# Cutting POOL's subtractions for the low parts of the weights into pieces of 256 columns

## The chip, the cores and the metric

The kernel runs on one core of one Trainium2 chip. The time is that of one execution on the device, in microseconds (us). A core has five engines that run their own instruction streams and meet at semaphores: TensorE (PE: matmuls, with weight loads counted beside them), VectorE (DVE), ScalarE (ACT), GpSimd (POOL) and SyncE (SP, which here only issues DMAs).

## What is computed

Attention with a window and four sink positions, then two mixtures of experts in a row. Cut to what matters here:

```python
x = attention(q, k, v)                      # 3072 tokens, 512 wide
# first mixture: each token goes to its best expert
h = np.maximum(x[mask] @ w1[e], 0.0)        # 512 -> 1024
out[mask] = gate_w[mask, None] * (h @ w2[e])
# second mixture: each expert takes 384 tokens, by a greedy assignment over all scores
for idx in np.argsort(-logits.flatten()):
    tok, e = idx // E, idx % E
    if assigned[tok] < 0 and counts[e] < cap: assigned[tok] = e; counts[e] += 1
h = np.maximum(x[mask] @ w1[e], 0.0)
out[mask] = h @ w2[e]
```

There are 8 experts in each mixture, with their own w1 (512 x 1024) and w2 (1024 x 512).

## The kernel before

Every product runs as three products of rounded numbers: each operand is split in a high part (ACT's cast to fp32r) and a low part (operand minus high part), and TensorE adds high x high, low x high and high x low. So each weight matrix of an expert needs a cast by ACT and a subtraction. Both work on a matrix in four parts (WP = 4) of 128 x 1024; w1 in parts of one row block each, w2 in parts of two.

The first mixture (324 to 728 us) runs over tiles of 128 tokens, ordered by expert; three experts have tokens here. DVE makes the low parts of w1 (low_w1, line 1413), POOL those of w2 (low_w2, line 523). POOL also gathers each tile's rows by an indirect DMA (line 515), two tiles ahead. For expert 0 POOL's order is: gather tiles 0 and 1, four w2 parts, gather tile 2. At a change of expert ACT casts w1, then scales the last tile's result, then casts w2, and POOL's four w2 parts stand in its queue ahead of the next gather. TensorE's up product waits for w1's parts one after the other.

The second mixture (728 us to the end) runs over 8 experts of 384 tokens. Here POOL makes all low parts. Its queue for expert k, written out by hand:

- for each of the eight blocks f of the hidden layer, low_h (line 586), which waits for ACT's two relus of that block; after each of the first four also one part of w2 (low_w2)
- the gather of the next expert's tokens (line 561, three indirect DMAs); w1 parts 0 and 1 of the next expert (low_w1, line 575), w1 part 2; the scatter of result tile 0 (line 592); low_x 0 (line 581), w1 part 3, low_x 1; a wait until the scatter has landed, scatter 1, low_x 2; the same wait, scatter 2, and a last wait.

TensorE computes the up product of block f (line 922 to 924) when ACT is done with block f-2 (two PSUM banks), and ACT's block f needs POOL's low_h of block f-2 (two h32 buffers). After eight blocks come three tiles of the down product (line 938 to 940), with the transposes of the next expert's gathered rows among them (line 753). The next expert's up product starts with a wait for all three low_x (line 912) and for w1's parts (line 921).

The second routing (the greedy assignment, rewritten as a search over thresholds) runs two experts ahead: DVE prepares `passed` (line 1509), TensorE counts with many small matmuls (line 833) that are placed among the products of experts 0 to 4 at fixed places, the first of them right behind an expert's first three products; experts 5 to 7 have none of it but a few leftovers of slots. DVE keeps one operand of nearly all its routing instructions in PSUM.

SP loads the raw w2 of the next expert when w2's four low parts are done, and raw w1 when those of w1 are.

Of the kernel before, what the change touches and what calls it, by code (L numbers as in the profile page):

```python
# [5 lines left out]
ALU = mybir.AluOpType  # L6
ACT = mybir.ActivationFunctionType
AX = mybir.AxisListType
F32 = mybir.dt.float32
# [9 lines left out]
def attention_then_two_moes(nc, qT, kT, v, mod_id, mod_bias, wg1, w1a, w2a, wg2, w1b, w2b, out):  # L19
# [5 lines left out]
    DM, E = wg1.shape  # L25
    F = w1a.shape[2]
    DC, FC = DM // P, F // P
# [24 lines left out]
    with ctx:  # L52
        def sb(name, shape, dt=F32):
            return ctx.enter_context(nc.sbuf_tensor("sb_" + name, shape, dt))
# [4 lines left out]
        def sem(name):  # L59
            return ctx.enter_context(nc.semaphore(name))  # L60
# [136 lines left out]
        w1h, w1l = sb("w1h", [P, DC, F], F32R), sb("w1l", [P, DC, F], F32R)  # L197
        w2h, w2l = sb("w2h", [P, FC, DM], F32R), sb("w2l", [P, FC, DM], F32R)
# [90 lines left out]
        w1_hi, w1_lo = [sem(f"w1_hi{m}") for m in range(2)], [sem(f"w1_lo{m}") for m in range(2)]  # L289
        w2_hi, w2_lo = [sem(f"w2_hi{m}") for m in range(2)], [sem(f"w2_lo{m}") for m in range(2)]  # L290
# [14 lines left out]
        WP = 4  # L305
        raw1, raw2 = w1_raw, w2_raw

        def w1_part(w, p):
            return w[:, p]

        def w2_part(w, p):
            return w[:, p * (FC // WP):(p + 1) * (FC // WP)]
# [110 lines left out]
        def _(pool):  # L423
# [96 lines left out]

            def low_w2(m, j, p):
                pool.wait_ge(w2_hi[m], j * WP + p + 1)
                pool.tensor_tensor(w2_part(w2l, p), w2_part(raw2, p), w2_part(w2h, p).bitcast(F32), ALU.subtract  # L523
                                   ).then_inc(w2_lo[m], 1)

            gather_x(0)
            gather_x(1)
            for p in range(WP):
                low_w2(0, 0, p)
            used = used_experts(pool)  # L530
            with pool.Fori(0, used) as e:
                first, end = order_of(pool, e, FIRST, END)
                with pool.Fori(first, end) as t:
                    gather_x(t + 2)
                first, end = order_of(pool, e + 1, FIRST, END)
                with pool.If(end > first):
                    for p in range(WP):
                        low_w2(0, e + 1, p)
# [33 lines left out]

            def low_w1(k, p):
                pool.wait_ge(w1_hi[1], k * WP + p + 1)
                pool.tensor_tensor(w1_part(w1l, p), w1_part(raw1, p), w1_part(w1h, p).bitcast(F32), ALU.subtract  # L575
                                   ).then_inc(w1_lo[1], 1)

            def low_x(k, i):
                pool.wait_ge(x2_hi, k * CT + i + 2)
# [21 lines left out]
            for p in range(WP):  # L601
                low_w1(0, p)
# [5 lines left out]
            def expert(k, a, last):  # L608

                for f in range(FC):  # L610
                    low_h(k, f)
                    if f < WP:
                        low_w2(1, k, f)

                if not last:
                    gather(k + 1, 1 - a)
                    low_w1(k + 1, 0)
                    low_w1(k + 1, 1)
                    keep_tokens(k + 1, 1 - a)
                    low_w1(k + 1, 2)  # L620
                scatter(k, a, 0)
                if not last:
                    low_x(k + 1, 0)
                    low_w1(k + 1, 3)
                    low_x(k + 1, 1)
                landed(k, 0)
                scatter(k, a, 1)
                if not last:
                    low_x(k + 1, 2)
                landed(k, 1)  # L630
                scatter(k, a, 2)
                landed(k, 2)
# [1024 lines left out]
```

## Time and profile before

| | |
|---|---|
| timed runs (3) | 1199.67, 1208.88, 1211.93 us; median 1208.88 |
| profiled execution | 1197.59 us, of it 1195.8 us span |
| busy | PE 1043.4, DVE 492.8, ACT 459.8, POOL 489.2 us |
| granted TensorE clock, mean | 0.925 of full speed |

The profile is of one execution. It has, among others, a view of groups of instructions by line, a timeline of single instructions, stretches with each engine's busy time and the granted TensorE clock, the waits, and the chain of work that ended last. In a timeline row the bracket tells how long the engine was idle before the instruction and what ended that. A matmul's duration is modelled and overlaps the next; the distance of two starts is what one costs. The full clock is 2.4 GHz and stands as 1.00; 0.50 is 1.2 GHz.

### The profile page before, as it was taken

What the parts mean: (1) busy time and instruction counts of PE and PEld (TensorE: products, weight loads), DVE (VectorE), ACT (ScalarE), POOL (GpSimd) and SP (SyncE); (2) the same over time, 40 slices, a digit from 0 to 9 for tenths busy, and PEclk for the clock granted to TensorE, in tenths of its full rate; (3) what the DMA queues carried; (4) which work ended last, traced back from release to release, by engine and by line L of the source; (5) the groups of instructions that cost most, each with busy time, mean ns of one, the idle gap of its engine ahead of it and who ended that gap; (6) DMA issues with size and microseconds to landing.
All of it is one profiled execution on the core that took longest, in us unless ns stands there. A gap on an engine that the chain in (4) does not pass through costs nothing.

```text
span 1195.8 us, 22961 instructions
## 1 busy us (share of the span) xinstructions
PE 1043.4 (87%) x7189; PEld 881.2 (74%) x7190; DVE 492.8 (41%) x1577; ACT 459.8 (38%) x1094; POOL 489.2 (41%) x453
## 2 busy tenths in 40 slices
PE   5999999999159999989999985259999999998796
PEld 4888888888147888878888874248777787887685
DVE  4566666665641111141112235864546455541000
ACT  4666666665032222242222240114243333433541
POOL 6443443442032000023000130226776766878782
PEclk9999999999569999999999997559898999988998
DMA  7545545642153111114111110322332333324300
GB/s 199 138 112 144 141 115 138 151 114 72 54 188 110 39 35 36 43 35 167 43 35 35 36 34 18 142 97 85 111 99 98 122 137 130 98 97 166 125 27 27
DMA packets 57148, 113.54 MB, mean 95 GB/s; under 512 B 6416, under 2 KB 22800, under 8 KB 57104
## 3 DMA queue, kind: packets, MB, share of 16 engines
q1 hardware_dynamic: 51024, 92.95, 25.6%
q0 software_dynamic: 6080, 19.98, 5.2%
q8 instruction: 31, 0.51, 0.2%
q14 instruction: 13, 0.11, 0.0%
HBM read 91.34 MB, written 21.57 MB: 94 GB/s over the span
## 4 chain that ended last, share of the span: by engine, by line
PE 48%; POOL 15%; issue 14%; DVE 8%; DMA 7%; ACT 4%; DVEq 2%; POOLq 1%; another core or an unknown queue 0%; SPq 0%; ACTq 0%
DMA out<-sb_rows_out,sb_tokens_at 5%; POOL sb_w2l L523 5%; PE ps_bank L792 4%; POOL sb_hl L586 4%; PE ps_bank L794 4%; PE ps_bank L793 4%; PE ps_bank L776 4%; PE ps_bank L774 4%; PE ps_bank L775 4%; PE ps_bank L677 3%; PE ps_bank L696 3%; PE ps_bank L694 3%; PE ps_bank L693 2%; PE ps_bank L712 2%; PE ps_bank L666 2%
## 5 line engine op out<-in xcount | busy, mean ns | idle before, releaser
L512 POOL COPY sb_gather_at<-sb_slot_token_i 128x1 int32 (+1 forms) x28 | 6.0, 214 | 329.9 <-PE ps_bank L753 275.5
L1424 DVE TENSOR_TENSOR sb_hl<-ps_bank,sb_hh 128x512 fp32r<-128x512 f32 x52 | 35.7, 686 | 231.9 <-ACT sb_hh L1049 231.9
L488 POOL TENSOR_TENSOR sb_kl<-sb_k_raw,sb_kh 128x768 fp32r<-128x768 f32 x32 | 58.3, 1821 | 148.0 <-ACT sb_kh L997 147.8
L981 ACT ACTIVATE sb_probs<-sb_masked,sb_neg_max 128x260 f32<-128x260 f32 (+1 forms) x192 | 94.0, 490 | 59.1 <-DVE sb_neg_max L1165 57.7
L523 POOL TENSOR_TENSOR sb_w2l<-sb_w_raw,sb_w2h 128x1024 fp32r<-128x1024 f32 x44 | 107.5, 2449 | 19.2 <-ACT sb_w2h L1035 14.0
L922 PE MATMUL ps_bank<-sb_xh,sb_w1h 128*128 128x384 f32 x256 | 99.3, 388 | 10.5 <-ACT sb_h L1104 7.8
L575 POOL TENSOR_TENSOR sb_w1l<-sb_w_raw,sb_w1h 128x1024 fp32r<-128x1024 f32 x32 | 75.6, 2377 | 39.5 <-ACT sb_w1h L1030 39.4
L1165 DVE CUSTOM_DVE_ANT_0 sb_masked<-ps_bank,sb_mask 128x260 f32<-128x260 f32 (+1 forms) x192 | 74.2, 399 | 42.4 <-PE ps_bank L666 37.0
L923 PE MATMUL ps_bank<-sb_xl,sb_w1h 128*128 128x384 f32 x256 | 91.3, 357 | 0.0
L774 PE MATMUL ps_bank<-sb_w1h,sb_xh 128*128 128x512 f32 x208 | 83.9, 403 | 8.1 <-DVE sb_w1l L1413 6.2
L924 PE MATMUL ps_bank<-sb_xh,sb_w1l 128*128 128x384 f32 x256 | 90.8, 355 | 0.0
L792 PE MATMUL ps_bank<-sb_w2h,sb_hh 128*128 128x512 f32 x208 | 86.5, 416 | 3.9 <-POOL sb_w2l L523 0.3
L833 PEld LDWEIGHTS ps_bank<-sb_choice,sb_passed 128*40 128x40 bf16 (+1 forms) x1344 | 46.0, 107 | 54.0 <-DVE sb_passed L1509 27.0
L938 PE MATMUL ps_bank<-sb_w2h,sb_hh 128*128 128x512 f32 x192 | 83.0, 432 | 0.0
L776 PE MATMUL ps_bank<-sb_w1h,sb_xl 128*128 128x512 f32 x208 | 83.0, 399 | 0.0
L775 PE MATMUL ps_bank<-sb_w1l,sb_xh 128*128 128x512 f32 x208 | 82.9, 399 | 0.0
L833 PE MATMUL ps_bank<-sb_choice,sb_passed 128*40 128x8 bf16 (+1 forms) x1344 | 53.8, 178 | 33.1 <-DVE sb_passed L1509 32.1
L677 PE MATMUL ps_bank<-sb_ident,sb_probs 128*128 128x128 f32 x352 | 76.3, 291 | 6.7 <-ACT sb_probs L981 5.2
L1103 ACT ACTIVATE sb_hh<-ps_bank 128x384 fp32r<-128x384 f32 x64 | 31.4, 491 | 130.7 <-PE ps_bank L924 109.2
L793 PE MATMUL ps_bank<-sb_w2l,sb_hh 128*128 128x512 f32 x208 | 81.2, 390 | 0.0
L794 PE MATMUL ps_bank<-sb_w2h,sb_hl 128*128 128x512 f32 x208 | 81.2, 390 | 0.0
L586 POOL TENSOR_TENSOR sb_hl<-sb_h,sb_hh 128x384 fp32r<-128x384 f32 x64 | 64.4, 1012 | 36.3 <-ACT sb_h L1104 35.9
(297 smaller groups left out, 2658.6 us busy)
## 6 DMA issues: line engine op xcount, KB each, us to landing
sb_w_raw<-w1b SPq DMA_DIRECT2D x8, 2048.0 KB, 8.7
sb_w_raw<-w2b SPq DMA_DIRECT2D x8, 2048.0 KB
sb_q_raw<-qT SPq DMA_DIRECT2D x64, 192.0 KB, 3.7
sb_k_raw<-kT SPq DMA_DIRECT2D x64, 192.0 KB, 4.0
y_rows<-sb_y_out SPq DMA_DIRECT2D x34, 258.0 KB, 2.5
sb_v<-v_tiles SPq DMA_DIRECT2D x32, 192.0 KB, 2.3
x_rows<-sb_x_pair SPq DMA_DIRECT2D x16, 384.0 KB, 4.3
sb_w_raw<-w1a SPq DMA_DIRECT2D x3, 2048.0 KB, 7.8
```

The lines of the kernel that those rows point to most:

```text
L523: pool.tensor_tensor(w2_part(w2l, p), w2_part(raw2, p), w2_part(w2h, p).bitcast(F32), ALU.subtract).then_inc(w2_lo[m], 1)
L586: pool.tensor_tensor(hl[:, f], h32[f % 2][:], hh[:, f].bitcast(F32), ALU.subtract).then_inc(h2_lo, 1)
L677: mm = pe.transpose(t[:, c * P:(c + 1) * P], probs[g % 2][:, at:at + P], ident[:])
L774: pe.matmul(hp, xh[:, c, 0:P], w1h[:, c, cols], start=(c == 0), stop=False)
L775: pe.matmul(hp, xh[:, c, 0:P], w1l[:, c, cols], start=False, stop=False)
L776: mm = pe.matmul(hp, xl[:, c, 0:P], w1h[:, c, cols], start=False, stop=(c == DC - 1))
L792: pe.matmul(y_ps[:], hh[:, f, 0:P], w2h[:, f], start=(f == 0), stop=False)
L793: pe.matmul(y_ps[:], hh[:, f, 0:P], w2l[:, f], start=False, stop=False)
L794: mm = pe.matmul(y_ps[:], hl[:, f, 0:P], w2h[:, f], start=False, stop=(f == FC - 1))
L833: mm = pe.matmul(r_ps[0:TRIES[s], 0:E], passed[:, t, 0:TRIES[s]], choice2[:, :, t], start=(t == 0), stop=(t == MT - 1))
L922: pe.matmul(hp, w1h[:, c, cols], xh[:, c], start=(c == 0), stop=False)
L981: act.activation(probs[g % 2][:, 0:width(g)], masked_scores[g % 2][:, 0:width(g)], ACT.Exp, bias=neg_max[g % 2][:], scale=-1.0, accum_out= ...
```

## The change

The two helpers that make POOL's low parts issue four subtractions of 256 columns for each part instead of one of 1024. The waits ahead of a part and the semaphore raised behind it stay: the last piece raises it. The same elements are computed in the same order, on the same engine, at the same place of its queue. DVE's low_w1 of the first mixture (line 1413) stays whole.

```diff
             def low_w2(m, j, p):
                 pool.wait_ge(w2_hi[m], j * WP + p + 1)
-                pool.tensor_tensor(w2_part(w2l, p), w2_part(raw2, p), w2_part(w2h, p).bitcast(F32), ALU.subtract
-                                   ).then_inc(w2_lo[m], 1)
+                low, raw, high = w2_part(w2l, p), w2_part(raw2, p), w2_part(w2h, p).bitcast(F32)
+                half = DM // 2
+                for f in range(FC // WP):
+                    for c in range(2):
+                        cols = slice(c * half, (c + 1) * half)
+                        op = pool.tensor_tensor(low[:, f, cols], raw[:, f, cols], high[:, f, cols], ALU.subtract)
+                op.then_inc(w2_lo[m], 1)
...
             def low_w1(k, p):
                 pool.wait_ge(w1_hi[1], k * WP + p + 1)
-                pool.tensor_tensor(w1_part(w1l, p), w1_part(raw1, p), w1_part(w1h, p).bitcast(F32), ALU.subtract
-                                   ).then_inc(w1_lo[1], 1)
+                low, raw, high = w1_part(w1l, p), w1_part(raw1, p), w1_part(w1h, p).bitcast(F32)
+                quarter = F // 4
+                for c in range(4):
+                    cols = slice(c * quarter, (c + 1) * quarter)
+                    op = pool.tensor_tensor(low[:, cols], raw[:, cols], high[:, cols], ALU.subtract)
+                op.then_inc(w1_lo[1], 1)
```

## Rows read from the trace of the kernel before

**Rows 1.** The page: TensorE's and POOL's busy times; the chain's shares by engine.

```profile
PE 1043.4 (87%) x7189; PEld 881.2 (74%) x7190; DVE 492.8 (41%) x1577; ACT 459.8 (38%) x1094; POOL 489.2 (41%) x453
...
PE 48%; POOL 15%; issue 14%; DVE 8%; DMA 7%; ACT 4%; DVEq 2%; POOLq 1%; another core or an unknown queue 0%; SPq 0%; ACTq 0%
```

**Rows 2.** Stretches: window, length, busy by engine, granted clock, DMA share, GB/s.

```profile
796.00:1056.00 260.00, 246.69 (x2091) 198.78 (x2092) 141.28 (x423) 96.30 (x164) 184.32 (x148) 0.94 0.33 112
```

**Rows 3.** Timeline into expert 5: start, duration, engine, line, operation, [idle before].

```profile
1055.09 1.28 POOL L581 TENSOR_TENSOR sb_xl<-sb_x,sb_xh 128x512 fp32r<-128x512 f32 x1
...
1056.42 0.45 PE L922 MATMUL ps_bank<-sb_xh,sb_w1h 128*128 128x384 f32 x1
```

**Rows 4.** POOL's groups by shape: count, busy us, mean ns, idle before, releasers.

```profile
L575 POOL TENSOR_TENSOR sb_w1l<-sb_w_raw,sb_w1h 128x1024 fp32r<-128x1024 f32 x32 | 75.6, 2377 | 39.5 <-ACT sb_w1h L1030 39.4
L586 POOL TENSOR_TENSOR sb_hl<-sb_h,sb_hh 128x384 fp32r<-128x384 f32 x64 | 64.4, 1012 | 36.3 <-ACT sb_h L1104 35.9
...
L489 POOL TENSOR_TENSOR sb_kl<-sb_k_raw,sb_kh 128x24 fp32r<-128x24 f32 x32 | 7.1, 223 | 0.0
```

**Rows 5.** Timeline of POOL, expert 1: two parts back to back.

```profile
888.79 4.72 POOL L575 TENSOR_TENSOR sb_w1l<-sb_w_raw,sb_w1h 128x1024 fp32r<-128x1024 f32 x2
```

**Rows 6.** Timeline of tile 0; the last row is of the chain.

```profile
352.77 9.40 POOL L523 TENSOR_TENSOR sb_w2l<-sb_w_raw,sb_w2h 128x1024 fp32r<-128x1024 f32 x4 [5.23 <-DMA sb_x_in<-x_rows,sb_gather_at]
...
362.23 0.50 PE L792 MATMUL ps_bank<-sb_w2h,sb_hh 128*128 128x512 f32 x1 [0.34 <-POOL sb_w2l L523]
...
363.10 7.81 DMA sb_x_in<-x_rows,sb_gather_at
```

**Rows 7.** DVE's w1 parts (ns minimum/median/maximum), then the timeline at a change of expert.

```profile
L1413 DVE TENSOR_TENSOR sb_w1l<-sb_w_raw,sb_w1h x12: 1215/1220/3405, 338.4 to 708.2; 128x1024 fp32r<-128x1024 f32 x12
...
534.10 2.89 POOL L523 TENSOR_TENSOR sb_w2l<-sb_w_raw,sb_w2h 128x1024 fp32r<-128x1024 f32 x1 [6.98 <-ACT sb_w2h L1035]
...
534.67 3.40 DVE L1413 TENSOR_TENSOR sb_w1l<-sb_w_raw,sb_w1h 128x1024 fp32r<-128x1024 f32 x1
...
538.13 0.50 PE L774 MATMUL ps_bank<-sb_w1h,sb_xh 128*128 128x512 f32 x1 [2.36 <-DVE sb_w1l L1413]
```

**Rows 8.** Stretches (columns as in group 2), for the granted clock.

```profile
538.50:541.50 3.00, 3.00 (x9) 2.37 (x8) 0.00 (x0) 0.60 (x1) 3.00 (x2) 0.53 0.64 182
...
856.00:862.00 6.00, 6.00 (x33) 5.10 (x32) 0.86 (x6) 1.80 (x3) 1.47 (x4) 0.51 0.32 126
1008.00:1012.00 4.00, 2.48 (x39) 1.88 (x40) 3.29 (x8) 0.59 (x1) 0.00 (x0) 1.00 0.94 372
...
1116.00:1126.00 10.00, 7.20 (x38) 6.25 (x38) 0.00 (x0) 3.55 (x7) 10.00 (x7) 1.00 0.00 0
```

**Rows 9.** Timeline, second mixture to expert 4: waits of POOL and TensorE.

```profile
780.54 0.19 POOL L556 COPY sb_slots_at<-sb_slots_i 128x3 int32<-128x3 int32 x1 [2.55 <-DVE sb_slots_i L1594]
...
883.23 1.01 POOL L586 TENSOR_TENSOR sb_hl<-sb_h,sb_hh 128x384 fp32r<-128x384 f32 x1 [2.54 <-ACT sb_h L1104]
...
907.34 0.68 PE L922 MATMUL ps_bank<-sb_xh,sb_w1h 128*128 128x384 f32 x1 [2.52 <-issue]
...
1010.14 0.57 PE L833 MATMUL ps_bank<-sb_choice,sb_passed 128*41 128x8 bf16 x16 [1.52 <-DVE sb_passed L1509]
...
1035.01 1.01 POOL L586 TENSOR_TENSOR sb_hl<-sb_h,sb_hh 128x384 fp32r<-128x384 f32 x1 [2.16 <-ACT sb_h L1104]
```

**Rows 10.** Timeline, experts 5 to 7: waits of POOL and TensorE.

```profile
1102.36 1.28 POOL L581 TENSOR_TENSOR sb_xl<-sb_x,sb_xh 128x512 fp32r<-128x512 f32 x1 [0.64 <-ACT sb_x L1096]
...
1136.60 1.11 PE L753 MATMUL ps_bank<-sb_ident,sb_rows_in 128*128 128x128 f32 x4 [4.21 <-DMA sb_rows_in<-y_rows,sb_slots_at]
...
1151.21 0.99 POOL L592 DMA_INDIRECT out<-sb_rows_out,sb_tokens_at  x1 [1.06 <-ACT sb_rows_out L1110]
...
1166.17 0.44 PE L922 MATMUL ps_bank<-sb_xh,sb_w1h 128*128 128x384 f32 x1 [0.94 <-ACT sb_h L1104]
```

**Rows 11.** DVE's `passed` in the second routing: ns minimum/median/maximum of 56.

```profile
L1509 DVE SCALAR_TENSOR_TENSOR sb_passed<-ps_bank,sb_edges,sb_tries x56: 876/882/887, 737.7 to 1040.9; 128x640 bf16<-128x640 f32 x56
```

## The prediction

> **What bounds the kernel now.** Look first at the page's busy times and at its chain of waits [rows 1]. TensorE is busy for 87% of the span, POOL for 41%, yet POOL has 15% of the chain. Read by stage, that is one stage: the second mixture of experts, from 797 us on, where POOL is busy for 184 of the 260 us of experts 0 to 4 [rows 2]. So I went through that stage boundary by boundary. TensorE can't start expert k+1 before POOL has written the last low part of its tokens (L581). Into expert 5 that part ends at 1056.37 and TensorE starts at 1056.42 [rows 3]; the other six boundaries are as close, or have another wait on top, named below. From POOL's eighth low_h to that part POOL hardly waits, and its four w1 parts lie in between. POOL is thus tied with TensorE at each boundary: what it gets slower comes out there, unless TensorE is held by something else.
>
> Before 725 us POOL is mostly idle, with three exceptions: tile 0 and the two changes of expert, below.
>
> **What one part costs in pieces.** A part is 1024 columns and becomes four of 256. POOL's rows of the same operation [rows 4]: 24 columns 0.223 us, 384 columns 1.012, 1024 columns 2.377. From 384 to 1024 that is 2.13 ns a column, from 24 to 384 it is 2.19; both lines give 0.73 for 256 columns. Queued back to back, two parts take 4.72 where their durations sum to 4.76 [rows 5], so the next starts 0.03 to 0.04 before the end. Four pieces: 3 x 0.695 + 0.73 = 2.82. The part gets 0.44 us dearer, four parts 1.74. Bounds: with the smaller slope and 0.05 of overlap 0.38 a part; with no overlap and small gaps (pieces of 0.75) 0.62 a part, 2.5 for four. There are 76 parts, so POOL gets some 33 us busier; the question is how much of that is in TensorE's way.
>
> By the Trainium skill (GPSIMD Engine Reference, section 3.1) a two-input elementwise operation costs about 2.6 cycles an element at 1.2 GHz and 4497 ns for 2048 columns; the fixed cost left is an estimated 0.06 us, four parts get 0.7 dearer, and the sum below would be near +1 and not +7. The row of 24 columns, 0.223 us, says that the fixed cost is near 0.17, so I go by the rows.
>
> **First mixture.** Tile 0: POOL does its four w2 parts from 352.77 to 362.17, TensorE waits 0.34 for the last of them at 362.23, and the gather queued behind them (363.10, landing 7.8 later) is what its next transposes wait for [rows 6]. All three move with POOL: +1.7.
>
> Changes of expert: here DVE and POOL are in each other's way. DVE's subtraction (L1413) of two SBUF tensors takes 1.22 at the median; two of the twelve show 3.4, exactly those that start while POOL's first w2 part runs. At 534.67 DVE's fourth w1 part starts and isn't done before 538.07, POOL's first part (from 534.10, 2.89) ends at 536.99. TensorE waits 2.36 for DVE's [rows 7]. Each holds what both need until its instruction ends. With pieces, POOL's first one begins to work when DVE's third is done, 534.75, and lets go 0.6 later, at 535.4; DVE's fourth is done at 536.6 in place of 538.07. That is 1.5 saved at each of two changes, -3.0. POOL's own parts end 1.7 later, at about 546.7, and the gather behind them is wanted a tile (20 us) later: nothing.
>
> TensorE's clock falls to 1.2 GHz (0.5 of full) after this wait: granted 0.53 from 538.5 to 541.5 [rows 8]. Seven matmuls then stand 0.43 apart where 0.23 is usual, 1.4 lost at each change. With a wait of 0.9 that may not happen: of the waits of about 1.5 us for DVE's `passed` one was followed by the low clock (0.51 from 856 to 862) and one wasn't (1.00 from 1008 to 1012) [rows 8]. I take half: -1.4. First mixture: +1.7 - 3.0 - 1.4 = -2.7.
>
> **Second mixture, experts 0 to 4 (with routing).** The four w1 parts of expert 0 come before a wait of 2.6 for DVE's slots [rows 9]: hidden. In each expert the four w2 parts stand among low_h 0 to 3, and POOL then waits for ACT before low_h 6 and 7: 2.54 before the eighth in expert 1, and nearly as much before the seventh; in expert 4 only before the eighth, 2.16 [rows 9]. TensorE needs low_h(f) only four blocks of f later. So 1.7 vanish there, and 3.4 (with the 1.7 left from the boundary before) do too in experts 1 to 3. The four w1 parts behind low_h 7 put the last token part 1.7 later, and TensorE with it, but the first four boundaries have cover: at three of them, into experts 1, 3 and 4, TensorE waits 1.5 for DVE's `passed` right behind its first three products (1.52 at 1010.14), and at the loop's turn, into expert 2, it stands still for 2.52 [rows 9]. DVE's chain hangs on ranks that TensorE delivered long before, so it doesn't shift. Loss: about 0.1 in all. If that cover were gone, each of the four would cost 1.1 to 1.7.
>
> Expert 4 has the least room: POOL arrives 1.4 late, adds 1.7, and has 2.2 of waiting: 0.9 remain, then 1.7 for the w1 parts. The boundary to expert 5 has no routing step and no slack: **+2.5**.
>
> **Experts 5 to 7 (no routing).** Here TensorE runs behind POOL: it waits for ACT, ACT for low_h, and at the transposes of expert 6 it waits 4.21 (in expert 5 nearly as much) for gathered rows that POOL issues after low_h 7 [rows 10]. Each group of four parts counts in full, less POOL's own waits. POOL's lateness: 2.6 into expert 5; w2 4.3; w1 6.1, less 0.64 that it waited before the last token part: 5.4; expert 6: w2 7.2, w1 8.9; expert 7: less 1.06 that it waited for ACT's copy [rows 10]: 7.9; three of the four w2 parts come before the low_h that releases TensorE's last block: **9.2**. After that TensorE works alone to the end.
>
> **Sum.** +9.2 - 2.7 = +6.5, and 1 for the clock (below): +7.5. It is made on the profiled execution, 1195.8 of span in 1197.59, which is below all three timed runs (1199.67 to 1211.93, median 1208.88). I put the difference on the median: **1216.4**, 0.6% above.
>
> **Rivals.**
> 1. *Dearer pieces, or the clock falls in the last experts.* Between its blocks TensorE idles up to 0.94 in expert 7 and is busy 7.2 of 10 us in expert 6, at full clock [rows 8, 10]. With POOL's pace of 3.75 a block instead of 3.3 it idles about 1.6. If the clock falls, products of 0.23 take 0.43, as from 856 on (six us at 0.51) [rows 8], and some 3 us are lost in expert 7, where nothing hides it. With 2.5 for four parts the covers of 1.5 no longer hold and the second mixture costs 15. Either gives +11 to +16, both +20: 1220 to 1228. Chance 0.27.
> 2. *Hidden.* If POOL's pieces overlap more than whole parts do, and four parts cost only 0.7, the slack in expert 4 takes them, and the same walk gives +2.4 behind, -2.3 to -3.7 in front: 1208. Against it: the 0.04 of overlap is the same for every pair in the trace. Chance 0.13.
> 3. *Faster.* The mechanism is the held port at the two changes of expert: 1.5 of wait and 1.4 of low clock saved at each, -5.8 with +1.7 for tile 0. It decides if the second mixture costs under 4, which by the walk means four parts under 1.1 dearer, a piece under 0.66. 1205 to 1207. By the Trainium skill (SBUF — State Buffer, Who interferes with whom) DVE with two SBUF inputs and POOL share one port and whoever is second blocks for the whole instruction; the 3.40 and 2.89 agree. If that rule also bit in the second routing, pieces would free DVE there. But DVE's `passed` takes 0.876 to 0.887 in all 56 cases, beside POOL's parts or not [rows 11]: there one input lies in PSUM, and nothing is to be freed. Chance 0.10.
>
> **Numbers.** Forecast 0.50, rivals 0.27, 0.13, 0.10. The range takes in rival 2 and most of rival 1, widened by the spread of the runs before: 1206 to 1228. A measurement of this kernel tells about 1% (12 us) from no change. The forecast stays inside it, rival 1 mostly goes over it, rival 3 reaches it only if DVE gains where I see nothing: faster 0.03, same 0.71, slower 0.26.
>
> **What would show it.** L523 and L575 at four times the count, 0.73 each. DVE's longest w1 part near 1.9, TensorE's wait there near 0.9. Boundaries 0 to 4 with the same starts after `passed`; the one to expert 5 with a wait of 2.5; low_h in experts 5 to 7 every 3.75 us. I would be wrong if a piece takes over 0.8 or under 0.66, if `passed` is late at the boundaries, or if the clock in experts 6 and 7 leaves 1.0.

## The result, and the profile after

| | before | after |
|---|---|---|
| median of 20 runs each | 1203.30 us (1194.74 to 1214.29) | 1209.94 us (1202.77 to 1219.08) |
| ratio after / before | | 1.0074, 95% interval 1.0049 to 1.0099 |
| profiled execution | 1197.59 us | 1207.53 us |
| POOL busy | 489.2 us | 521.0 us |
| granted TensorE clock, mean | 0.925 | 0.927 |

The kernel is slower by 0.74%, 8.9 us (0.0074 x 1203.3; the interval is 6 to 12 us; the two medians lie 6.6 apart). The ratios here and below leave out executions more than 1.5% above the fastest of their kernel. Forecast was +7.5 us, 0.6%. The difference is surely there, yet under the 1% that the chances were given for.

The page after, first the busy times, then the chain's shares. Beside [rows 1] POOL has 31.8 us more work, TensorE's is the same, and POOL's share of the chain went from 15% to 21%.

```profile
PE 1044.9 (87%) x7189; PEld 881.9 (73%) x7190; DVE 490.7 (41%) x1577; ACT 459.3 (38%) x1094; POOL 521.0 (43%) x681
...
PE 45%; POOL 21%; issue 10%; DMA 8%; DVE 7%; ACT 3%; DVEq 1%; POOLq 1%; ACTq 0%
```

To see where the time went I cut each trace at the same instructions: the first up product of the first mixture, the first up product of each expert of the second mixture, and the start of the last down product (line 940 before, 949 after). All times in us.

| stage | before | after | difference |
|---|---|---|---|
| first mixture to expert 0 (with the routing's start) | 450.20 | 446.94 | -3.3 |
| experts 0 to 4 | 258.93 | 260.36 | +1.4 |
| expert 5 | 48.03 | 49.63 | +1.6 |
| expert 6 | 45.17 | 49.93 | +4.8 |
| expert 7, to the last product | 34.87 | 36.16 | +1.3 |
| sum | 837.20 | 843.02 | +5.8 |

The spans differ by 9.8 us. 4.0 of them lie ahead of the first up product (347.29 and 351.32), in attention, whose code is the same. So single executions are compared stage by stage, and the total by the timed runs. (A stage of one trace scatters too: in the five traces below and before whose first mixture has whole parts and the routing as it was, it takes 448.23 to 451.12.)

The price of a piece, first from the groups by shape (count | busy us, mean ns), then from the timeline (start, duration): 0.728 us a piece, and four of them in 2.80 us where a part took 2.38 [rows 4]. The mean of the w2 pieces, 754 ns, holds a few of the first mixture that stood beside DVE's work, up to 1.72; their median is 0.734.

```profile
L528 POOL TENSOR_TENSOR sb_w2l<-sb_w_raw,sb_w2h 128x256 fp32r<-128x256 f32 x176 | 126.4, 754 | 19.5 <-ACT sb_w2h L1044 14.0 <-DMA sb_x_in<-x_rows,sb_gather_at 5.5
L584 POOL TENSOR_TENSOR sb_w1l<-sb_w_raw,sb_w1h 128x256 fp32r<-128x256 f32 x128 | 89.1, 728 | 38.2 <-ACT sb_w1h L1039 38.0
...
822.01 2.80 POOL L528 TENSOR_TENSOR sb_w2l<-sb_w_raw,sb_w2h 128x256 fp32r<-128x256 f32 x4
```

At a change of expert in the first mixture (compare [rows 7]) DVE's longest w1 part is down from 3.40 to 1.76, and TensorE's wait for it from 2.36 to 0.71. The view of DVE's line (ns minimum/median/maximum), and the timeline:

```profile
L1422 DVE TENSOR_TENSOR sb_w1l<-sb_w_raw,sb_w1h x12: 1215/1219/1760, 342.6 to 711.8; 128x1024 fp32r<-128x1024 f32 x12
...
542.66 0.51 PE L783 MATMUL ps_bank<-sb_w1h,sb_xh 128*128 128x512 f32 x1 [0.71 <-DVE sb_w1l L1422]
```

In the second mixture TensorE now waits for POOL's last low part of the tokens at each of its seven boundaries. Before, the view of waits had no such line. Waits of TensorE after (sum, count, longest), and two of the seven in the timeline:

```profile
PE ps_bank L931 <- POOL sb_xl L590: 9.6, 7, 1.9
...
854.64 0.44 PE L931 MATMUL ps_bank<-sb_xh,sb_w1h 128*128 128x384 f32 x1 [1.75 <-POOL sb_xl L590]
1058.62 0.44 PE L931 MATMUL ps_bank<-sb_xh,sb_w1h 128*128 128x384 f32 x1 [1.92 <-POOL sb_xl L590]
```

In the last experts the pieces set TensorE's pace: two blocks of expert 6 start 3.72 us apart, each behind ACT's copy, which waits for low_h. The last row is TensorE's wait for the gathered rows in expert 6, which POOL asks for after its eighth low_h.

```profile
1122.97 0.44 PE L931 MATMUL ps_bank<-sb_xh,sb_w1h 128*128 128x384 f32 x1 [1.36 <-ACT sb_h L1113]
1126.69 0.45 PE L931 MATMUL ps_bank<-sb_xh,sb_w1h 128*128 128x384 f32 x1 [1.35 <-ACT sb_h L1113]
...
1143.51 0.90 PE L762 MATMUL ps_bank<-sb_ident,sb_rows_in 128*128 128x128 f32 x3 [4.56 <-DMA sb_rows_in<-y_rows,sb_slots_at]
```

### The profile page after: what moved, and what is told of

It reads as the page before. It is cut to its first block, busy times and chain, and to the rows that moved or that the text cites. A ratio compares the mean times of both kernels' runs of the same rounds, so it can differ in the third digit from the quotient of the medians.

```text
span 1205.6 us, 23189 instructions
## 1 busy us (share of the span) xinstructions
PE 1044.9 (87%) x7189; PEld 881.9 (73%) x7190; DVE 490.7 (41%) x1577; ACT 459.3 (38%) x1094; POOL 521.0 (43%) x681
## 4 chain that ended last, share of the span: by engine, by line
PE 45%; POOL 21%; issue 10%; DMA 8%; DVE 7%; ACT 3%; DVEq 1%; POOLq 1%; ACTq 0%
POOL sb_w2l L528 8%; DMA out<-sb_rows_out,sb_tokens_at 6%; POOL sb_w1l L584 5%; PE ps_bank L801 4%; POOL sb_hl L595 4%; PE ps_bank L686 4%; PE ps_bank L705 4%; PE ps_bank L802 3%; PE ps_bank L803 3%; PE ps_bank L785 3%; PE ps_bank L783 3%; PE ps_bank L784 3%; PE ps_bank L703 3%; PE ps_bank L702 3%; DMA sb_x_in<-x_rows,sb_gather_at 2%
## 5 line engine op out<-in xcount | busy, mean ns | idle before, releaser
L528 POOL TENSOR_TENSOR sb_w2l<-sb_w_raw,sb_w2h 128x256 fp32r<-128x256 f32 x176 | 126.4, 754 | 19.5 <-ACT sb_w2h L1044 14.0
L584 POOL TENSOR_TENSOR sb_w1l<-sb_w_raw,sb_w1h 128x256 fp32r<-128x256 f32 x128 | 89.1, 728 | 38.2 <-ACT sb_w1h L1039 38.0
L842 PE MATMUL ps_bank<-sb_choice,sb_passed 128*40 128x8 bf16 (+1 forms) x1344 | 53.9, 178 | 29.3 <-DVE sb_passed L1518 28.6
L1068 ACT ACTIVATE sb_y_out<-ps_bank,sb_slot_gate 128x512 f32<-128x512 f32 x26 | 17.9, 688 | 159.2 <-PE ps_bank L803 159.2
```

Of the source, the lines that this page charges most:

```text
L528: op = pool.tensor_tensor(low[:, f, cols], raw[:, f, cols], high[:, f, cols], ALU.subtract)
L584: op = pool.tensor_tensor(low[:, cols], raw[:, cols], high[:, cols], ALU.subtract)
L842: mm = pe.matmul(r_ps[0:TRIES[s], 0:E], passed[:, t, 0:TRIES[s]], choice2[:, :, t], start=(t == 0), stop=(t == MT - 1))
```

## The experiments

The theory: two effects of opposite sign. Four pieces cost POOL 1.7 us more than four parts, which comes out in the second mixture; they release DVE at the two changes of expert in the first. The rivals put the loss elsewhere (the clock, the last two experts alone), or see no gain in front. All eleven kernels below were each compared with the kernel before on the same chip. Diffs are against the kernel after unless said otherwise.

### One mixture alone

The pieces only in the second mixture. There `low_w2_cut` is the helper after, `low_w2` the whole one:

```diff
-                        low_w2(1, k, f)
+                        low_w2_cut(1, k, f)
```

> The kernel after, but with the first mixture's w2 parts whole again. Theory (a part costs 0.44 us more in pieces; in the second mixture that comes out at the boundaries and in experts 5 to 7, and the first mixture gives 2.7 to 3 back): the loss without the gain, +9 us on the kernel before, 1.0075, DVE's two w1 parts of 3.4 us are there again, and from the first up product of expert 0 to the last product TensorE takes 9 us longer than before. Rival A (the loss is where low clock happens to fall, not POOL's price): the second mixture's length differs by under 3 us and the lateness appears elsewhere. Rival B (attention, 4 us later in the profile after, has its part): the same 4 us before the first tile.

The pieces only in the first mixture, all of the second mixture's parts whole:

```diff
-                low_w2(0, 0, p)
+                low_w2_cut(0, 0, p)
...
-                        low_w2(0, e + 1, p)
+                        low_w2_cut(0, e + 1, p)
```

> Pieces in the first mixture alone. Theory: +1.7 for tile 0, and at each of the two changes of expert 1.5 for the port that is let go earlier and 1.4 for the clock that stays up: -3 to -4 us on the kernel before, 0.997; TensorE's wait for DVE's fourth w1 part 0.7 in place of 2.4. Rival A: the clock falls all the same, then -1.3 and nothing that a run can tell.

| kernel | ratio to before | first mixture to expert 0 | second mixture |
|---|---|---|---|
| before | 1 | 450.20 | 387.00 |
| after | 1.0074 (1.0049 to 1.0099) | 446.94 | 396.08 |
| second alone | 1.0089 (1.0049 to 1.0129) | 451.12 | 398.36 |
| first alone | 0.9946 (0.9914 to 0.9977) | 446.68 | 383.87 |

The two signs are shown. +0.89% and -0.54% sum to +0.35%, the whole change measured +0.74%; the intervals of the two (0.4 and 0.3 to either side) allow both. In the trace of the second alone DVE's longest part is back at 3.398 us; in that of the first alone the first mixture is as short as after. Rival B is out: the first up product starts at 352.68 and 354.88 in these two traces, later than after (351.32), and the first alone is the faster kernel all the same.

Of the first alone's -6.5 us by the timed runs the trace shows -3.5 where its code differs. Another 3.1 are in the second mixture, whose code is that of before. Counting the clock that was not granted in experts 0 to 4 (the sum of 1 minus the granted clock over stretches of 1 us) gives 15.6 us before and 12.7 here; what is left is 243.3 and 242.9. So in this trace those 3 us are clock.

The same split can be made of every timed run, since each lists its span and its mean granted clock. Span times clock is what is left at full clock, span times (1 - clock) is the clock that was not granted. For the first alone the means are 1104.8 and 89.2 us, for the kernel before on the same chip 1104.3 and 95.2. So the whole gain of the first alone is clock that was granted, 6.0 us with a standard error of 1.6; the waits that it shortens and the dearer tile 0 cancel. The two changes of expert explain 3 of these 6 us (worked out further down, under *First mixture*). Where the others lie, or if they are chance, is not shown. For the second alone the loss is in the other part: 1114.7 against 1104.3. All kernels are in a table behind the experiments.

### The last two experts alone

```diff
-            def expert(k, a, last):
+            def expert(k, a, last, cut=False):
+                w1, w2 = (low_w1_cut, low_w2_cut) if cut else (low_w1, low_w2)
...
-            expert(E - 2, 0, False)
-            expert(E - 1, 1, True)
+            expert(E - 2, 0, False, True)
+            expert(E - 1, 1, True, True)
```

> Pieces only in the last two experts of the second mixture: 12 of the 76 parts. Theory: no routing covers anything there, so w2 of expert 6 (+1.7), w1 of expert 7 (+1.7), and three quarters of w2 of expert 7 (+1.3) less 1.06 that POOL waited come out in full: +3.7 us, 1.003, from 12 parts; experts 0 to 5 unchanged. Rival (the price spreads evenly, 9.2 us over 76 parts): +1.4 us.

Ratio 1.0013 (0.9979 to 1.0048): the ratio can't tell a loss of 3.7 us from one of 1.4 (and the medians lie 5.4 apart). With the clock taken out the timed runs can: 1108.8 against 1104.3, +4.5 with a standard error of 0.6, so these 12 parts cost what the theory says and far more than their share by count. In the trace experts 0 to 5 took 306.82 (before 306.96), expert 6 took 48.94 (+3.8) and expert 7 35.83 (+1.0). The window of expert 6 (length, busy by engine, granted clock) says that not all of the 3.8 is POOL's pace: the clock of expert 6 was 0.93, against 0.96 over the same stretch before, which is 3.4 and 1.8 us not granted. About 1.6 of the 3.8 may be that. The row is that of expert 6:

```profile
1111.13:1160.07 48.94, 37.83 (x182) 32.44 (x180) 0.00 (x0) 19.86 (x34) 40.13 (x54) 0.93 0.29 103
```

### Taking turns in place of pieces

If the gain in front is the held port alone, whole parts must give it too as soon as POOL doesn't start beside DVE. Parts whole everywhere, and at a change of expert POOL waits for DVE's fourth w1 part:

```diff
                 with pool.If(end > first):
+                    pool.wait_ge(w1_lo[0], e * WP + 3 * WP)
                     for p in range(WP):
                         low_w2(0, e + 1, p)
```

> The kernel before, whole parts, but at a change of expert POOL waits for DVE's last w1 part before it starts its first w2 part. Theory (DVE and POOL hold what both need until an instruction ends): DVE's four parts take 1.22 each, the last is done at 535.9 in place of 538.1, 2.2 us saved at each change, and the clock stays up, 1.4 more: -4.4 to -7.2 us on the kernel before, 0.994 to 0.996, with nothing to pay in the second mixture. POOL's four parts take 9.4 and not 10.9. Rival (what saved time was the smaller pieces, not the order): nothing gained, since POOL starts 1.8 us later and something waits for it.

Ratio 0.9925 (0.9893 to 0.9958): faster than both kernels. The first mixture took 443.49, 6.7 less than before and 3.5 less than with the pieces, which keep the dearer tile 0 and a rest of the blocking. No DVE part is longer than 1.227 us, and TensorE's wait for the fourth is 0.17. POOL starts when DVE is done, at 545.27, and its four parts are still in time (in all of this trace TensorE waits for one of them once, 0.2 us). The second mixture took 384.60, 2.4 less than before with the same code, again by the clock (in experts 0 to 4 12.9 not granted against 15.6; the rest 243.2 against 243.3). By the timed runs 2.8 of the gain are there at full clock and 4.9 are clock (standard errors 0.8 and 1.9), so here, other than with the pieces, the waits give something too.

```profile
L1414 DVE TENSOR_TENSOR sb_w1l<-sb_w_raw,sb_w1h x12: 1212/1218/1227, 347.2 to 713.8; 128x1024 fp32r<-128x1024 f32 x12
...
545.14 0.50 PE L775 MATMUL ps_bank<-sb_w1h,sb_xh 128*128 128x512 f32 x1 [0.17 <-DVE sb_w1l L1414]
545.27 9.42 POOL L523 TENSOR_TENSOR sb_w2l<-sb_w_raw,sb_w2h 128x1024 fp32r<-128x1024 f32 x4 [8.94 <-ACT sb_w2h L1036]
```

### Other widths

The same change with pieces of 512 columns, and with 128:

```diff
-                    for c in range(2):
-                        cols = slice(c * half, (c + 1) * half)
+                    for c in range(DM // 512):
+                        cols = slice(c * 512, (c + 1) * 512)
...
-                for c in range(4):
-                    cols = slice(c * quarter, (c + 1) * quarter)
+                for c in range(F // 512):
+                    cols = slice(c * 512, (c + 1) * 512)
```

> All 76 parts in two pieces of 512 columns. Theory (every instruction more costs 0.145 us, whatever its width): a piece takes 1.28, a part 0.15 more, four parts 0.6; the room before low_h 6 and 7 and behind the boundaries takes that in experts 0 to 4, experts 5 to 7 add some 2 us; DVE's fourth w1 part is freed after 1.15 in place of 2.3, 1.1 saved at each change, and the clock may stay up: +2 +0.6 -2.2 and 0 to -2.8, that is -2.4 to +0.5 us, 0.998 to 1.000. Rival (the price goes with the bytes or with the first cut, not with the count): as after, 1.007.

> All 76 parts in eight pieces of 128 columns. Theory: a piece takes 0.46, the next starts 0.04 before its end, a part takes 3.4 in place of 2.38, four parts 4.1 more, 8.2 an expert. POOL has some 6 us of waiting an expert in experts 0 to 4 and 1 behind: what is over that comes out, +25 to +35 us, 1.02 to 1.03, and TensorE waits for POOL's last low_x at every boundary. Rival (a walk by 256 columns scaled up with no regard to the room, 9.2 us for 0.44 a part): +21 us.

| width | mean of one | a part | first mixture | second mixture | ratio |
|---|---|---|---|---|---|
| 1024 | 2.377 | 2.38 | 450.20 | 387.00 | 1 |
| 512 | 1.279 | about 2.52 | 445.99 | 387.60 | 0.9967 (0.9933 to 1.0001) |
| 256 | 0.728 | 2.80 | 446.94 | 396.08 | 1.0074 (1.0049 to 1.0099) |
| 128 | 0.451 | about 3.3 | 454.88 | 425.08 | 1.0371 (1.0302 to 1.0441) |

(A part of 512 and of 128 is the mean times the count, less 0.04 for each overlap [rows 5].) Each instruction has a fixed price, and beside it one of 2.15 us for 1000 columns: from 1024 to 512 columns (2.377 - 1.279) / 512 = 2.14 ns a column, from 256 to 128 it is 2.16, which leaves 0.17 to 0.18 us fixed. At 512 columns the dearer parts fit in POOL's slack in experts 0 to 4, where TensorE's waits sum to 12.3 us against 11.8 before. They do not in the last three: expert 6 took 47.25, 2.1 more than before (up to 1.7 of it clock). The gain in front is there already. But the ratio is not told from 1, and it is the clock's doing: at full clock the timed runs are 3.8 us longer than before (standard error 0.7), and the clock not granted is 8.4 less (2.2).

At 128 I missed: +45 us by the ratio (0.0371 x 1204.4; 43 by the medians) where 25 to 35 were expected. Two steps were left out. The down products of the first mixture now wait for POOL's w2 parts (second line), and in the second mixture all experts, those with routing too, go at POOL's pace, 53.9 to 54.9 us each for experts 1 to 6. The waits of TensorE on POOL:

```profile
PE ps_bank L929 <- POOL sb_xl L588: 25.8, 7, 4.1
PE ps_bank L799 <- POOL sb_w2l L527: 7.3, 7, 1.6
```

### The routing's operand in SBUF

The third rival turned on whether DVE's `passed` is untouched by POOL because one of its inputs is in PSUM. Here `value` is moved to SBUF, once with whole parts and once with pieces:

```diff
+        value_sb = sb("value", [P, MT])
...
-        score_ps, value_ps = scratch_cols(0, MT * E), scratch_cols(MT * E, MT)
+        score_ps, value_ps = scratch_cols(0, MT * E), value_sb[:, :]
```

> The kernel before with one tile of the second routing, the value that DVE compares with its thresholds, in SBUF and not in PSUM, so that DVE's `passed` reads two SBUF tensors; whole parts. Theory (DVE and POOL share what a second SBUF input goes through, and hold it for an instruction): `passed` isn't 0.88 each time any more but up to 3.3 where a part of POOL's runs, POOL's parts up to 3.3, the routing chain is late at the boundaries and at the counts, +5 to +20 us on the kernel before. Rival (only large subtractions get in each other's way, or only w1's own tiles): `passed` stays at 0.88 and the time is that of before.

> The same, value in SBUF, with all of POOL's parts in pieces of 256. Theory: `passed` waits at most a piece, its longest is 1.7; here the pieces give back what they cost: the time is below that of value_sbuf_whole by 0 to 10 us, though still above the kernel before. Rival (pieces can't help since POOL's next piece takes its turn first): `passed` up to 3.3 again and 9 us over value_sbuf_whole.

DVE's `passed`, ns minimum/median/maximum of 56, whole and then in pieces (before 876/882/887 [rows 11]):

```profile
L1510 DVE SCALAR_TENSOR_TENSOR sb_passed<-sb_value,sb_edges,sb_tries x56: 875/889/3075, 752.2 to 1079.8; 128x640 bf16<-128x640 f32 x56
```

```profile
L1519 DVE SCALAR_TENSOR_TENSOR sb_passed<-sb_value,sb_edges,sb_tries x56: 872/912/1635, 749.5 to 1065.7; 128x640 bf16<-128x640 f32 x56
```

With both inputs in SBUF one `passed` takes up to 3.08 beside whole parts, 1.42 in the mean, and up to 1.64 beside pieces, 1.09 in the mean. With the input in PSUM it is 0.88 beside either. So of the forms tried the blocking is there for two SBUF inputs alone, and `passed` had nothing to gain from the pieces because `value` lies in PSUM. The ratios are 1.0202 (1.0135 to 1.0270) with whole parts and 1.0263 (1.0189 to 1.0337) with pieces. In the two traces experts 0 to 4 go from 280.03 to 274.78 with the pieces, and from the first up product to the last product it is 865.85 and 859.50; the timed runs, four of each, lie the other way, and their intervals overlap. With the clock taken out the timed runs agree with the traces (1127.4 with whole parts, 1123.0 with pieces, standard error of the difference 1.4); what turns the order round is clock, 103 us not granted against 112. That the instruction gets shorter is shown. That the program gains by it is not.

### One matrix alone

First w1 in pieces and w2 whole, which leaves the first mixture as it was; then w2 of the second mixture in pieces and all else whole:

```diff
-                low, raw, high = w2_part(w2l, p), w2_part(raw2, p), w2_part(w2h, p).bitcast(F32)
...
+                pool.tensor_tensor(w2_part(w2l, p), w2_part(raw2, p), w2_part(w2h, p).bitcast(F32), ALU.subtract
+                                   ).then_inc(w2_lo[m], 1)
```

```diff
-                        low_w2(1, k, f)
+                        low_w2_cut(1, k, f)
...
-                low, raw, high = w1_part(w1l, p), w1_part(raw1, p), w1_part(w1h, p).bitcast(F32)
...
+                pool.tensor_tensor(w1_part(w1l, p), w1_part(raw1, p), w1_part(w1h, p).bitcast(F32), ALU.subtract
+                                   ).then_inc(w1_lo[1], 1)
```

> Of all parts only POOL's w1 parts of the second mixture in pieces; w2 whole in both mixtures. Theory (walk of the prediction with the w2 terms left out): every boundary 1.7 later on POOL, hidden at the first four; +1.7 into expert 5, +1.1 to 1.7 into 6, +1.7 into 7, less 1.06 that POOL waits there: +3.5 to 5 us. Rival (w1 parts sit right before the boundary, so they carry all of the loss and the w2 parts vanish among low_h): the whole +9 to +11.

> Only POOL's w2 parts of the second mixture in pieces. Theory: nothing in experts 0 to 4, since POOL waits 2.2 to 5 us there before low_h 6 and 7; +1.7 in expert 5, +1.7 in expert 6, +1.3 in expert 7: +4 to +5 us. Rival as for w1_only: under 1 us.

w1 alone 1.0050 (1.0008 to 1.0092), w2 alone 1.0029 (0.9993 to 1.0066); together +0.79%, and the second mixture alone gave +0.89%. At the boundaries the two differ as the queue says they should. With w1 in pieces TensorE waits for the tokens' low parts at six of them; with w2 in pieces, whose 1.7 us go into POOL's waits for ACT, at one, for 0.4 (the line is that of w1).

```profile
PE ps_bank L926 <- POOL sb_xl L585: 9.3, 6, 1.9
```

In experts 5 to 7, without routing, both count: 3.5 more than before for w1, 5.1 for w2. With the clock taken out of the timed runs w1 alone costs 5.5 us, w2 alone 6.1, and both, the second mixture alone, 10.4. So the rival of both expectations, that w1 carries all and w2 vanishes, is out.

### Turns, and DVE for the last w2

DVE is idle in experts 6 and 7. On top of the kernel that takes turns, DVE makes the low parts of w2 for these two:

```diff
-                    if f < WP:
+                    if f < WP and not (isinstance(k, int) and k >= E - 2):
                         low_w2(1, k, f)
...
+            for k in (E - 2, E - 1):
+                for p in range(WP):
+                    dve.wait_ge(w2_hi[1], k * WP + p + 1)
+                    dve.tensor_tensor(w2_part(w2l, p), w2_part(raw2, p), w2_part(w2h, p).bitcast(F32), ALU.subtract
+                                      ).then_inc(w2_lo[1], 1)
```

> As turns (whole parts, POOL waits for DVE at a change of expert), and DVE, which has nothing left to do after the last slots, makes the w2 low parts of experts 6 and 7. Theory (experts 6 and 7 go at POOL's pace): TensorE's blocks there come every 2.1 us and not every 3.3, expert 6 takes some 40 us in place of 45.1, expert 7 some 31.5 in place of 34.9: 6 to 9 us below turns, 0.985 to 0.988 of the kernel before. DVE's and POOL's subtractions there block each other, up to 2.2 us each. Rival (they only take turns at the same port, nothing is won): as turns, 0.9925.

Ratio 0.9865 (0.9829 to 0.9901), the fastest of all, 1186.09 us at the median, by six executions. The place of the gain was only half right. Expert 6 took 42.84, 2.3 less than with turns alone, expert 7 32.89, 2.0 less: smaller than expected. In expert 6 POOL's w1 parts for expert 7 bound it next, with 1.09 of wait at the boundary. Another 5.6 us of this trace lie in experts 0 to 4, whose code is unchanged: 7.9 us of clock not granted against 12.9, rest 242.6 against 243.2. DVE needs 1.35 us for a part at the median and up to 2.08 where POOL works beside it:

```profile
L1631 DVE TENSOR_TENSOR sb_w2l<-sb_w_raw,sb_w2h x8: 1225/1349/2084, 1099.7 to 1148.9; 128x1024 fp32r<-128x1024 f32 x8
```

### The timed runs with the clock taken out

Means over the executions that the ratios use; differences are to the kernel before on the same chip, with their standard errors. Over the 34 executions of before on one chip a microsecond of clock not granted lengthened the span by 0.78 and not by 1 (a straight line through them), so that taking it out whole takes a little too much. The kernel after has no such pair on record; its 20 executions have 1112.8 and 95.8 us. The four kernels that are faster than before all have 4.9 to 8.4 us less clock not granted, which is more than the two changes of expert explain.

| kernel | at full clock | difference | clock not granted | difference |
|---|---|---|---|---|
| before, on three chips | 1104.3, 1103.2, 1103.0 | | 95.2, 99.0, 96.0 | |
| second alone | 1114.7 | +10.4 (1.1) | 97.0 | +1.7 (2.1) |
| first alone | 1104.8 | +0.5 (0.5) | 89.2 | -6.0 (1.6) |
| last two experts | 1108.8 | +4.5 (0.6) | 94.6 | -0.6 (1.7) |
| turns | 1101.5 | -2.8 (0.8) | 90.3 | -4.9 (1.9) |
| 512 columns | 1107.0 | +3.8 (0.7) | 90.6 | -8.4 (2.2) |
| 128 columns | 1132.7 | +29.5 (0.6) | 113.1 | +14.1 (3.0) |
| `value` in SBUF, whole | 1127.4 | +24.2 (1.2) | 103.1 | +4.1 (4.6) |
| `value` in SBUF, pieces | 1123.0 | +19.8 (0.8) | 111.8 | +12.8 (4.0) |
| w1 alone | 1108.5 | +5.5 (1.2) | 97.0 | +1.0 (2.9) |
| w2 alone | 1109.1 | +6.1 (0.7) | 97.2 | +1.2 (2.3) |
| turns, DVE for the last w2 | 1095.2 | -7.8 (1.2) | 90.1 | -5.9 (2.4) |

## Why the prediction held, point by point

**What bounds.** Right. POOL was tied with TensorE at each boundary of the second mixture. Its later end came out there, as seven waits where there were none.

**The price of a piece.** Right: 0.728 measured for 0.73, four pieces 2.80 for 2.82, POOL 31.8 us busier for 33. The estimate worked out from the Trainium skill's figures for two-input elementwise operations (GPSIMD Engine Reference, section 3.1), a fixed cost of 0.06 us by which four parts would get 0.7 dearer and the sum be near +1, falls: four parts got 1.7 dearer, and the kernel 8.9 us slower. The page's 2.6 cycles an element, 2.17 ns at 1.2 GHz, agree with the 2.14 to 2.16 ns a column measured here.

**First mixture.** Forecast -2.7, measured -3.3 in the trace after and -3.5 with the first mixture alone. By its terms, from POOL's starts at tile 0 and the two changes of expert:

- Tile 0: +1.7 forecast, +1.8 measured. From the first up product to POOL's first w2 part at the first change it is 186.81 before and 188.96 after; over all traces with whole parts there it is 186.6 to 187.6, mean 187.1, over three with pieces of 256 it is 188.7 to 189.1, mean 188.9. POOL's first parts are now waited for too: TensorE's down product at 368.24 waits 1.04, and the transposes at 377.12 wait 0.89 for the gather.
- The changes: 1.5 of wait saved and 0.7 of clock at each forecast, -4.4 in all; measured -2.53 and -2.64, -5.2 in all. (From POOL's start at the first change to that at the second it is 173.53 before and 171.00 after; from there to the routing's first use of the results 22.24 and 19.60.) How much of it is wait and how much clock was mis-sized both ways, and the traces settle it, since the clock did not always fall. From POOL's start at the first change to that at the second it takes 173.4 to 173.7 in the four traces with whole parts where the clock fell after the wait at the first change (before, second alone, w2 alone, `value` in SBUF), 172.1 and 172.0 in the two where it stayed up after the same wait (last two experts, w1 alone), and 170.9 to 171.0 in three with pieces of 256. So the clock is 1.5 a change and the shorter wait 1.1, though TensorE's wait for DVE went down by 1.65 (2.36 to 0.71). Where the other 0.6 comes back is not shown.

Taking half of the clock's 1.4 was a guess. Over all thirteen traces the low clock followed 10 of the 12 waits of 2.3 to 2.4 us behind whole parts, and none of the 14 changes where TensorE waited at most 1.26. So the sum, -3.3 for -2.7, is near in part by luck: the wait's term was too large by 0.4 a change, the clock's too small by 0.8. Without the clock hardly anything is gained: +1.8 for tile 0, -2.2 for the two waits, which goes with the timed runs of the first alone (+0.5 at full clock, standard error 0.5). First a stretch after, where before 0.53 stood [rows 8] (granted clock: third number from the end); then the first change with whole parts where the clock stayed up behind the full wait, in the trace of the last two experts alone:

```profile
540.00:547.00 7.00, 6.12 (x29) 4.50 (x30) 2.60 (x2) 4.24 (x7) 6.72 (x8) 1.00 0.51 174
...
546.40 0.50 PE L794 MATMUL ps_bank<-sb_w1h,sb_xh 128*128 128x512 f32 x1 [2.35 <-DVE sb_w1l L1433]
546.50:550.00 3.50, 3.50 (x16) 2.84 (x17) 0.00 (x0) 0.60 (x1) 3.50 (x2) 1.00 0.60 188
```

The Trainium skill's rule on the shared port (SBUF — State Buffer, Who interferes with whom) agrees with each reading here: 3.40 us for DVE beside whole parts, 1.76 beside pieces, 1.23 when they take turns, and 0.88 for `passed` with a PSUM input beside either. The last kernel's 2.08 fits as well.

**Experts 0 to 4.** Forecast: about 0.1 at the first four boundaries, and 2.5 into expert 5, 2.6 in all. Measured: +1.4 in the traces; with the clock taken out it is 243.3 before and 247.4 after, +4.1, and 2.7 came back as clock (12.9 us not granted against 15.6). All waits of TensorE in these experts sum to 11.8 us before and 15.6 after, +3.8, and they say where it is. At the five boundaries TensorE waits 8.3 for POOL, 1.1 to 1.9 each. In exchange the three waits of 1.5 for `passed` and the standing still at the loop's turn are gone, and 1.1 for `passed` is new there: +2.4, of it 1.9 into expert 5. So the cover did its work; it left 0.4 where I had 0.1, for a delay of 1.7 to 1.9 is a little more than a wait of 1.5. Another 0.9 are waits for ACT among the blocks of expert 4; with the 1.9 behind them they are the 2.5 that I had put into expert 5's boundary alone. The last 0.6, at the transposes for gathered rows, the walk had left out. With w1 alone in pieces the waits for POOL are 8.8 at the same five boundaries and the sum is only 1.5 above before (13.3), for which the walk gives 1.7. Into expert 2, the loop's turn, the 2.52 of standing still [rows 9] is gone and in its place are 1.11 for POOL and then 1.12 for DVE:

```profile
904.04 0.44 PE L931 MATMUL ps_bank<-sb_xh,sb_w1h 128*128 128x384 f32 x1 [1.11 <-POOL sb_xl L590]
...
905.94 0.70 PE L842 MATMUL ps_bank<-sb_choice,sb_passed 128*41 128x8 bf16 x15 [1.12 <-DVE sb_passed L1518]
```

**Experts 5 to 7.** The mechanism was right: pace 3.72 a block for 3.75, the gather waited for 4.42 and 4.56 at the transposes, full groups of four parts counted. Forecast +6.7 (9.2 less 2.5), measured +7.7, most of it in expert 6 (4.8). TensorE's waits there sum to 15.9 before and 22.8 after: +7.0, of it 2.3, 3.5 and 1.2 in the three experts. What expert 6 shows above its 3.5 is clock: 3.4 us not granted in it, 1.7 before. In expert 5 it is the other way round (3.4 and 6.8), which hides part of the loss there.

**The sum.** Second mixture +9.1 for +9.2 and 1 for the clock; first -3.3 for -2.7; total by the timed runs +8.9 for +7.5. The second mixture's closeness is in part luck: TensorE's waits grew by 10.8 where 9.2 were forecast, and the clock, which was to cost 1, gave some back (19.7 us not granted from the first up product of expert 0 on, 24.1 before). The 1 us for the clock is a term that no run shows: the timed runs of after have 95.8 us not granted, those of before 95.2 to 99.0.

**The rivals.** *Dearer pieces, or the clock falls*: refuted. A piece costs what was forecast, and in the up products of experts 6 and 7 the clock stayed at 1.00 though TensorE idles some 1.35 a block. It leaves 1.00 in expert 6 only about the wait for the gathered rows, as before, though for 6.8 us and not for 3.4:

```profile
1110.00:1136.00 26.00, 19.54 (x103) 17.68 (x102) 0.00 (x0) 11.65 (x22) 19.86 (x27) 1.00 0.21 75
1160.00:1180.00 20.00, 17.36 (x96) 16.41 (x95) 0.00 (x0) 10.07 (x19) 18.03 (x25) 1.00 0.03 13
```

*Hidden*: refuted at 256 columns. At 512 it holds in experts 0 to 4 and not in the last three: whether slack takes a dearer part is a matter of its size. *Faster*: the mechanism is real (first mixture alone 0.9946, by the clock that stays up), its condition isn't met, since the second mixture costs 9.1 and not under 4.

## What to carry to other kernels

Cutting an instruction that holds a shared port buys the other engine time and is paid for on each piece, here 0.15 us for each further one: weigh the pieces that lie on the critical path against the waits that they shorten. Where only two places collide, let the engines take turns there (0.9925) rather than cut everywhere (1.0074). A new wait is not yet a loss: look for the waits that it replaced (8.3 us of new waits for POOL cost 2.4). And where runs differ by less than a percent, split each span by its granted clock before naming a cause: here the whole gain of the pieces in front was clock.

## What the chip did that I had not expected

- The same code of experts 0 to 4, with whole parts, lost between 7.9 and 15.6 us to the low clock (15.6 before and with the last two experts cut, 12.7 with the first mixture alone, 12.9 with turns, 7.9 with DVE's last parts). With pieces there it was 12.9 after and 20.8 with w2 alone. With the clock taken out, the kernels with whole parts there agree within 0.7 (242.6 to 243.3). A difference of 3 us in one trace says nothing until this is taken out.
- The first up product of the first mixture starts between 347.3 and 357.2 us in eleven of these traces, behind unchanged attention code, and at 361.8 and 363.1 in both with `value` in SBUF. I didn't find out why, nor whether the move of that tensor does it.
- At the loop's turn between experts 1 and 2 TensorE stands still for 2.1 to 2.6 us in four traces (2.52 before, 2.35 with the last two experts cut, 2.07 with the first mixture alone, 2.61 with turns) and waits for nothing that the profile shows; with `value` in SBUF and whole parts it is 3.59. Where TensorE waits for POOL at this place, be it only for 0.4 (w2 alone) or 0.7 (DVE's last parts, whole parts there), the gap isn't there. Its cause stays open.
